# An attention, a dense layer and eight experts on one core: the first layer's tiles 0 and 1 begun inside the last pair of heads, and identity matmuls ahead of the first scores

## What is computed

```python
# attention over equal buckets, for 2 x 8 heads of 768 x 64
q_bucket = sum(((q @ proj) > 0) * powers)          # 6 bits; the same for k
scores = where(q_bucket == k_bucket, (q @ k.T) / 8, -1e9)
x = softmax(scores) @ v                            # -> 1536 tokens x 512
# first layer
h = maximum(x @ w_in, 0.0)                         # 512 -> 2048
x = (h * h) @ w_out                                # 2048 -> 512
# experts: w_gate gives logits; (token, expert) pairs are taken in order of size,
# at most 192 tokens for each of 8 experts; each token then goes through its expert
out[mask] = maximum(x[mask] @ w1[e], 0.0) @ w2[e]
```

## Time and profile before

| | us |
|---|---|
| median of 3 runs | 836.95 |
| lowest and highest | 836.59 and 838.42 |
| the profiled execution | 838.97 |
| its span, first to last instruction | 837.2 |
| TensorE busy | 783.4 (94%) |
| GpSimd busy | 398.9 (48%) |
| VectorE busy | 379.8 (45%) |
| ScalarE busy | 377.2 (45%) |

### The profile page before, as it was taken

How to read it: one execution, slowest core, us unless ns; L and a number is a source line. 1 busy time by engine, 2 the same in 40 slices (tenths; PEclk the granted TensorE clock), 3 DMA queues, 4 the chain that set the end, 5 groups by cost and what they waited for, 6 DMA issues and landing times. The chain is left out here.

```text
span 837.2 us, 14217 instructions
## 1 busy us (share of the span) xinstructions
PE 783.4 (94%) x4720; PEld 714.6 (85%) x4720; DVE 379.8 (45%) x875; ACT 377.2 (45%) x655; POOL 398.9 (48%) x326
## 2 busy tenths in 40 slices
PE   5999999999999799999999999984599999999986
PEld 3898898898887688999999999973499999999986
DVE  6576576576672443322232234224555345345500
ACT  2677777777676455545545554530012122212221
POOL 5567777777577576646656675640100110011001
PEclk9999999999999899999999999995599999999999
DMA  6564775875541000100000010010635455364541
GB/s 157 121 150 109 157 180 127 187 187 126 141 126 51 0 1 0 38 1 0 1 38 0 0 39 0 0 38 0 220 122 173 166 176 183 119 218 149 179 170 38
DMA packets 43687, 81.38 MB, mean 97 GB/s; under 512 B 17176, under 2 KB 17176, under 8 KB 43136
## 3 DMA queue, kind: packets, MB, share of 16 engines
q1 hardware_dynamic: 41440, 74.58, 31.5%
q0 software_dynamic: 2048, 6.29, 2.3%
q10 hardware_dynamic: 160, 0.00, 0.0%
HBM read 54.55 MB, written 6.29 MB: 73 GB/s over the span
## 5 line engine op out<-in xcount | busy, mean ns | idle before, releaser
L1122 PE MATMUL banks<-xt_hi,split_parts 128*128 128x384 f32 (+1 forms) x512 | 142.2, 339 | 0.2 <-POOL split_parts L886 0.2
L309 POOL TENSOR_TENSOR pt_lo<-pt,pt_hi 128x768 fp32r<-128x768 f32 x64 | 117.7, 1846 | 48.0 <-ACT pt_hi L438 38.4
L1133 PE MATMUL banks<-split_parts,h_hi 128*128 128x512 f32 x384 | 122.8, 401 | 5.7 <-DVE h_lo L1048 5.6
L886 POOL TENSOR_TENSOR split_parts<-w_in_sb,split_parts 128x512 fp32r<-128x512 f32 x64 | 84.4, 1319 | 91.1 <-ACT split_parts L879 89.8
L1045 DVE TENSOR_TENSOR h<-relu 128x384 f32<-128x384 f32 x64 | 43.6, 681 | 184.6 <-ACT relu L1000 184.6
L431 ACT ACTIVATE pt<-banks 128x768 f32<-128x768 f32 x96 | 78.1, 813 | 60.8 <-PE banks L683 54.2
L544 DVE TENSOR_REDUCE mx<-banks 128x1 f32<-128x768 f32 x96 | 90.5, 957 | 23.4 <-PE banks L710 19.5
L1566 PE MATMUL banks<-x_cols,w_in_sb 128*128 128x192 f32 x512 | 96.6, 342 | 1.1 <-ACT x_cols L1346 1.1
L1122 PEld LDWEIGHTS banks<-xt_hi,split_parts 128*128 128x128 f32 x512 | 94.3, 190 | 3.3 <-POOL split_parts L886 0.5
L1580 PE MATMUL banks<-expert_hidden,w_out_sb 128*128 128x192 f32 x512 | 94.0, 334 | 0.0
L890 POOL TENSOR_TENSOR split_parts<-w_out_sb,split_parts 128x512 fp32r<-128x512 f32 x64 | 84.2, 1315 | 16.2 <-ACT split_parts L882 16.2
(11 more groups left out here) (195 smaller groups left out, 1354.6 us busy)
## 6 DMA issues: line engine op xcount, KB each, us to landing
w_in_sb<-in_moe_w SPq DMA_DIRECT2D x8, 2048.0 KB, 9.7
w_out_sb<-in_moe_w SPq DMA_DIRECT2D x8, 2048.0 KB, 8.6
w_in_sb<-in_moe_w_in SPq DMA_DIRECT2D x8, 512.0 KB, 6.5
w_out_sb<-in_moe_w_out SPq DMA_DIRECT2D x8, 512.0 KB, 6.4
w_out_sb<-in_k SPq DMA_DIRECT2D x16, 192.0 KB, 3.7
w_out_sb<-in_q SPq DMA_DIRECT2D x16, 192.0 KB, 4.0
v_raw<-in_v SPq DMA_DIRECT2D x16, 192.0 KB, 3.4
ka<-split_parts SPq DMA_DIRECT2D x16, 192.0 KB, 3.0
```

The lines of the kernel that those rows point to most:

```text
L309: pool.tensor_tensor(pt_lo[x % 2][:], pt[j % 2][:], pt_hi[x % 2][:].bitcast(fp32), ALU.subtract).then_inc(los, 1)
L886: pool.tensor_tensor(wil[i], in_view(f), wih[i].bitcast(fp32), ALU.subtract).then_inc(wils, 1)
L1122: last = pe.matmul(PB[i][:, 0:HALF], w_[:, k, :], x_[:, xs], start=n == 0, stop=n == 3 * DT - 1)
L1133: last = pe.matmul(PB[2 + t][:], h_[:, tc], w_[:], start=start and n == 0, stop=stop and n == 2, skip_group_check=True)
```

## The change

It has these parts.

- The splits of the first weights go from the last pair of heads to the one before (`p + 2 == PAIRS`), spread between its steps. `weights(n)` runs for n = 2 to 9 (`w_in`) and 10 to 13 (`w_out`), one load in each half pair. ScalarE waits for nine loads, not twelve.
- `hidden` for tiles 0 and 1 goes into the last pair of heads on TensorE (`early_hidden`), behind `scores_t` 2 and 4 of head 15; relu and square (`tile`) stand in ScalarE's queue of the last pair.
- The last `sums`, `high`, `low` and `turn` of the attention go into the first layer's queues, behind or between its first steps (`later`).
- `project` does the products with high parts alone first, waits for the low part behind them, and `z_k`/`z_q` start on the high part.
- `keep_warm` on TensorE multiplies the identity by itself: nine matmuls of 128x384 before the first projection, three before `rows(0)`, four behind it.

```diff
-                if 4 <= n < 12:
-                    load_in(sp, n - 4)
-                if 9 <= n < 13:
-                    load_out(sp, n - 9)
+                if 2 <= n < 10:
+                    load_in(sp, n - 2)
+                elif 10 <= n < 14:
+                    load_out(sp, n - 10)
 # GpSimd, pair p
                     q_low(pool, p + 2)
+                if p + 2 == PAIRS:
+                    split["in_low"](pool, 0, 0, 0)
                 if p:
                     low(p - 1)
                 low_part(2 * p + 1, 1)
+                if p + 2 == PAIRS:
+                    split["in_low"](pool, 1, 1, 1)
                 low_part(2 * p + 1, 2)
+                if p + 2 == PAIRS:
+                    split["out_low"](pool, 0, 0, 0)
                 low_part(2 * p + 1, 3)
                 low_part(2 * p + 1, 4)
-                if p + 1 == PAIRS:
-                    split["in_low"](pool, 0, 0, 0)
-                    split["in_low"](pool, 1, 1, 1)
-                    split["out_low"](pool, 0, 0, 0)
...
-            low(PAIRS - 1)
+            later["low"] = lambda: low(PAIRS - 1)
 # ScalarE, pair p
-                if p + 1 == PAIRS:
-                    ...
-                    act.wait_ge(split["w_early"], 16 * 12)
-                    split["in_high"](act, 0, 0)
-                    split["in_high"](act, 1, 1)
-                    split["out_high"](act, 0, 0)
                 v_high(2 * p + 1, 1)
                 ...
                 q_high(p + 2)
+                if p + 2 == PAIRS:
+                    for taken in (ka_in, kb_in, qa_in, qb_in):
+                        act.wait_ge(taken[0], 32 * (PAIRS - 1) - (16 if taken in (kb_in, qb_in) else 0))
+                        act.wait_ge(taken[1], 32 * (PAIRS - 1))
+                    act.wait_ge(split["w_early"], 16 * 9)
+                    split["in_high"](act, 0, 0)
...
                 expo_high(2 * p + 1, 1)
+                if p + 2 == PAIRS:
+                    split["in_high"](act, 1, 1)
                 expo(2 * p + 1, 2)
                 expo_high(2 * p + 1, 2)
+                if p + 2 == PAIRS:
+                    split["out_high"](act, 0, 0)
...
                 expo(2 * p + 1, 4)
+                if p + 1 == PAIRS:
+                    split["tile"](act, 0, 0)
...
-            sums(HEADS - 1, 1)
-            high(PAIRS - 1)
+            split["tile"](act, 1, 1)
+            later["sums"] = lambda: sums(HEADS - 1, 1)
+            later["high"] = lambda: high(PAIRS - 1)
 # TensorE
-            def project(slot, hi, lo, done):
+            def project(slot, hi, lo, low, count, done):
                 for h in range(2):
                     c = slice(h * HALF, (h + 1) * HALF)
                     pe.matmul(slot[:, h, 0:HALF], p_hi[:], hi[:, c], start=True, stop=False)
-                    pe.matmul(slot[:, h, 0:HALF], p_hi[:], lo[:, c], start=False, stop=False)
-                    last = pe.matmul(slot[:, h, 0:HALF], p_lo[:], hi[:, c], start=False, stop=True)
+                    pe.matmul(slot[:, h, 0:HALF], p_lo[:], hi[:, c], start=False, stop=False)
+                pe.wait_ge(low, count)
+                for h in range(2):
+                    c = slice(h * HALF, (h + 1) * HALF)
+                    last = pe.matmul(slot[:, h, 0:HALF], p_hi[:], lo[:, c], start=False, stop=True)
...
+            def early_hidden(g):
+                if g == 0:
+                    pe.wait_ge(mxs, 6 * HEADS - 1)
+                    pe.wait_ge(xl, 5)
+                split["hidden"](pe, g, 0, g)
...
                 scores_t(2 * p + 1, 1, p, 2)
+                if last:
+                    early_hidden(0)
...
                 scores_t(2 * p + 1, 1, p, 4)
+                if last:
+                    early_hidden(1)
...
+            def keep_warm(slot, n):
+                for _ in range(n):
+                    pe.matmul(slot[:, 0, 0:HALF], identr[:], identr[:].unsqueeze(1).broadcast_to([P, 3, P]), start=True, stop=True)
+
+            keep_warm(PREP, 9)
             pe.wait_ge(proj_split, 1)
...
+            pe.wait_ge(mxs, 5)
+            keep_warm(PREP, 3)
             rows(0, 0)
+            keep_warm(PREP, 4)
             pair(0, 1, True, False)
 # first layer, GpSimd
             for g in range(6):
                 both_low(g, g + 2, g + 1, g % 2)
+                if g == 1:
+                    later["low"]()
 # first layer, ScalarE, first chunk
+                    in_high(2, 2, 0)
+                    out_high(1, 1, 1)
+                    later["sums"]()
+                    in_high(3, 3, 1)
+                    out_high(2, 2, 0)
+                    later["high"]()
                     for g in range(2, 8):
                         tile_high(g, g + 2, g + 1, g % 2)
 # first layer, VectorE, first chunk: tile j
                     hidden(c * FT + j, j % 2)
                     if first:
-                        if j == 1:
+                        if j < 2:
+                            later["divisors"](j)
+                        elif j == 3:
 # first layer, TensorE
-            hidden(0, 0, 0)
             chunk(0, 0, HALF, True, False)
```

More of the change, by code:

```diff
@@ L639, in _, with last_divisors @@
             pair(PAIRS - 1, 0, False, True)
[L641 to L644, removed]
+            def last_divisors(h):
+                turn(HEADS - 1, 1, h)
+                if h:
+                    reciprocals(HIGH)
+            later["divisors"] = last_divisors
         @block.tensor
@@ L839, in _ @@
             weigh_low(HEADS - 1, 1, 4, False, True)
+        return later
 def routing_constants(nc, ctx):
@@ L870, in weight_splits, with hidden, tile @@
     wihs, wils, wohs, wols = (sem("split_" + n) for n in ("wihs", "wils", "wohs", "wols"))
+    hid, relus, hhs = (sem("first_" + n) for n in ("hid", "relus", "hhs"))
+    r32 = [ctx.enter_context(nc.sbuf_tensor(f"relu{i}", [P, HALF], fp32)) for i in range(2)]
+    hh = [ctx.enter_context(nc.sbuf_tensor(f"h_hi{i}", [P, HALF], f32r)) for i in range(2)]
+    def hidden(pe, g, x0, i):
+        pe.wait_ge(wils, g + 1)
+        n = 0
+        for k in range(DT):
+            xs = bass.ds(x0 + k * S, HALF)
+            for w_, x_ in ((wih[i], xt_hi), (wih[i], xt_lo), (wil[i], xt_hi)):
+                last = pe.matmul(PB[i][:, 0:HALF], w_[:, k, :], x_[:, xs], start=n == 0, stop=n == 3 * DT - 1)
+                n += 1
+        last.then_inc(hid, 1)
+    def tile(act, g, i):
+        act.wait_ge(hid, g + 1)
+        act.activation(r32[i][:], PB[i][:, 0:HALF], ACT.Relu).then_inc(relus, 1)
+        act.wait_ge(relus, g + 1)
+        act.activation(hh[i][:], r32[i][:], ACT.Square).then_inc(hhs, 1)
     def in_view(f):
@@ L892, in weight_splits, with first_layer @@
     return dict(stage=stage, wih=wih, wil=wil, woh=woh, wol=wol, wihs=wihs, wils=wils, wohs=wohs, wols=wols, w_early=w_early, w_ready=w_ready,
-                in_high=in_high, out_high=out_high, in_low=in_low, out_low=out_low)
-def first_layer(nc, block, sem, PB, ident, K, finish, low_done, xt_hi, xt_lo, split, wg, L, stored, y_rows):
+                hid=hid, relus=relus, hhs=hhs, r32=r32, hh=hh, hidden=hidden, tile=tile, in_high=in_high, out_high=out_high, in_low=in_low, out_low=out_low)
+def first_layer(nc, block, sem, PB, ident, K, finish, low_done, xt_hi, xt_lo, split, wg, L, stored, y_rows, later, h32, hl):
     with ExitStack() as ctx:
@@ L1108, in _ @@
         def _(pe):
-            pe.wait_ge(split["w_early"], 16 * 12)
-            pe.wait_ge(split["w_ready"], 16 * 5)
+            pe.wait_ge(split["w_early"], 16 * 9)
+            pe.wait_ge(split["w_ready"], 16 * 8)
             pe.sem_inc(rows_done, 2)
             def hidden(g, x0, i):
-                pe.wait_ge(wils, g + 1)
-                if past(g, 2):
-                    pe.wait_ge(relus, g - 1)
-                n = 0
-                for k in range(DT):
-                    xs = bass.ds(x0 + k * S, HALF)
-                    for w_, x_ in ((wih[i], xt_hi), (wih[i], xt_lo), (wil[i], xt_hi)):
-                        last = pe.matmul(PB[i][:, 0:HALF], w_[:, k, :], x_[:, xs], start=n == 0, stop=n == 3 * DT - 1)
-                        n += 1
-                last.then_inc(hid, 1)
+                pe.wait_ge(relus, g - 1)
+                split["hidden"](pe, g, x0, i)
             def rows(g, i, start, stop):
@@ L1189, in chunk @@
                 if not last:
-                    pe.wait_ge(head_low, 1)
+                    if not first:
+                        pe.wait_ge(head_low, 1)
                     hidden(g0 + FT, x_next, 0)
@@ L1227, in experts @@
             K["weigh"], K["ones"], K["tri"], K["iota_j"], K["tabs"], K["masks"], K["lift"], K["pref"], K["ids"])
+        xg = [sb(f"x_rows{i}", [CH, 2, DM]) for i in range(2)]
+        xgt = sb("x_cols", [P, DT, CAP])
+        hs = sb("expert_hidden", [P, F2T, CAP])
+        oc = sb("expert_out_cols", [P, DT, CAP])
+        og = sb("expert_out", [CH, 2, DM])
         m = sb("best", [P, NT])
```

49 lines of the change are left out of this document (19 added, 30 removed).

## The result

| | before | changed |
|---|---|---|
| median of the runs, us | 837.32 (836.59 to 838.42, 4 runs) | 829.3 (827.04 to 830.64, 4 runs) |
| ratio | | 0.9889, 95% interval 0.9851 to 0.9927 |
| the profiled execution, its span | 838.97, 837.2 | 830.64, 828.9 |

The forecast was 829.9. The span fell by 8.3 us, where the terms of the forecast gave 7.1. The total is close. The reason given for its largest term was in good part not right, and one gain of 1.0 us has no term in it.

The account below looks back on a forecast made before the run. TensorE was taken as the bound: only its idling, low clock or added work counts. From 838.97 us, -8.8 (passage and pair 6) and +1.7 (front) give 831.9, less 2.0 for the median: 829.9; range 827.2 to 833.8.

Parts of the forecast that it names:

- What bounds the kernel: Whole kernel: TensorE is busy throughout full stretches, so time is lost only to its idling, lower clock or added work.
- Passage, 8.6 us removed: From attention to first layer: 0.20 and 5.63 us idle plus 2.75 us of low clock go, with h_lo ready.
- Filling the last pair, 1.3 us: Last pair of heads: the moved hidden groups fill part of its 1.45 us of TensorE idle time, gaining 1.3 us.
- New stalls, 0.8 us: First layer's start: hidden group 2 and rows group 2 wait on late GpSimd and VectorE steps, costing 0.8 us.
- Pair 6, 0.3 us: Pair 6: moved splits delay GpSimd's third low part of head 13 by about 1.1 us, costing 0.3 us.
- Weights' loads, nothing: Attention pairs: weights' loads, one each half pair from pair 1 instead of two from pair 2, cost nothing.
- The front, +1.7 us: Kernel start: warming gains 0, opens a gap of some 3 us before head 1's scores; the fallen clock costs 1.7 us.
- High parts first, nothing: Projections inside the loop: TensorE is full and low parts are ready long before, so the new order gains 0.
- A: Front: the clock holds through the gap; 828.2 us, or 827.5 with all gaps of the last pair filled; 25%.
- B: Passage and pair 6: new waits on GpSimd and VectorE queues replace the old one; 832.9 to 834.2 us; 20%.
- C: Attention from 29 us: the clock stays at 1.2 GHz, a whole pair giving 843.7 us, slower than before; 3%.
- D: Last pair: hidden group 0 waits inside it as long as it did behind it; 837 to 838 us; 2%.

Follow-up runs that it names:

- the kernel with hidden 0 and 1 behind: Changed kernel with the first two hidden groups after the attention's last matmul and their relu and square after its last exponential; 830.86 us.
- the kernel with the early splits alone: Kernel before with only the first weights' splits and the loads they need moved to pair 6; 830.9 us, ratio 0.99.
- the kernel with the filled gap: Changed kernel with fifteen more identity matmuls behind weigh(0, 0, 0), ahead of the scores of head 1; 825.38 us, ratio 0.9833.
- the one with the wait for the low part: Changed kernel with later q loads, no identity matmuls, and z_k and z_q waiting for the low part before their first matmul; 828.02 us.
- The front alone: Kernel before with only project, z_k, z_q and keep_warm of the changed kernel; 838.81 us, ratio 1.0012.

## Why the prediction came out right, step by step

One row of the trace of before bears on the first of the terms, the last `sums` of the attention on ScalarE:

```profile
273.98 0.81 ACT L448 ACTIVATE num<-banks 64x768 f32<-64x768 f32 x1 [6.66 <-POOL inverse L316]
```

- **What bounds the kernel.** Right: all that was won was idle time, low clock or (the layer's pace) length of TensorE's own work.
- **Passage, 8.6 us removed.** Right in size: no gap, no low clock. By the starts of TensorE's matmuls 9.1 us went: the last two of the attention to rows group 5 took 34.78 us (268.47 to 303.25) and now take 22.45 (273.48 to 295.93); 4.17 of the difference are the two moved groups, and 0.96 of new stalls (below) stand against the rest. The reason given was right in part: it named the attention's last `sums` and `high` ahead of the relu in ScalarE's queue. But it said that the gap goes because hidden 0 gets a head start in the last pair, and with hidden 0 behind the pair there was no gap either. The gap came from the order in two queues, and the forecast overlooked the first of them. GpSimd's three subtractions stood ahead of the divisions, ScalarE's `sums` waited for these, and the relu stood behind that (the earlier trace rows has the subtractions at 268.16, the divisions at 271.88 and VectorE's wait for the relu until 276.20; the row above has the 6.66 us that `sums` waited for the divisions). Out of the 9.1 us the passage gave at rows group 5, moving the splits to pair 6 gives 5.3, letting the attention's last steps go behind the first tiles' relu 3.0 (the difference to the kernel with hidden 0 and 1 behind), and the head start 0.7. The 9.1 is firm: less their lateness behind pair 6, the seven executions of kernels with all these parts reach rows group 5 9.0 to 9.1 us earlier than before.
- **Filling the last pair, 1.3 us.** The last two matmuls of the attention start at 268.47 in before. With the lateness of 1.74 and two hidden groups of 2.08 each (half of the changed kernel's 4.17 for a tile) they would start at 274.38 without a fill. They started at 273.48: 0.9 us. About half of it is the copies' departure, since the kernel with the early splits alone also got 0.46 us less late in this pair.
- **New stalls, 0.8 us.** Hidden 2 waited 0.50 for the row that was named, at the top of its 0.2 to 0.5; rows 2 came 0.17 late and rows 3 0.07. Together 0.74; by the starts, rows 0 to rows 3 take 13.47 us, 0.96 more than three tiles at 4.17. The price of VectorE's steps behaved as said: 1.49 us at 275.64 beside GpSimd at work, 0.56 at 273.84 in the kernel with hidden 0 and 1 behind, where GpSimd had nothing to do. The Trainium skill, "SBUF — State Buffer", section "SBUF: two separate sides", says that such a VectorE step and such a GpSimd instruction take one port pair in turn; this case's trace agrees (1.49 and 0.56 us).
- **Pair 6, 0.3 us.** 0.35 by the marks. The third low part was 1.0 us later than the lateness carried in, as forecast 1.1.
- **Weights' loads, nothing.** Right for the profiled execution: the lateness stays between 1.39 and 1.55 us from the first pair to the sixth. Other executions of kernels with the new loads show a wait for a transfer in the attention (last section).
- **The front, +1.7 us.** The mechanism was right: the scores stayed, a gap of 3.23 us opened, the clock fell and came back after 3.4 us. The cost was 1.5 us, of which the runs put 1.1 on the clock; 0.4 is that the queue's own end came later with the warming (29.13 to 29.46 in five executions, against 28.91 and 28.94 where TensorE waited without it). TensorE's work ahead of the gap ended at 26.05, where 25 to 26 was forecast, though the clock was down from 15.1 to 21.9 (last section). The Trainium skill, "TensorE: Matmul & The Clock Gate", section "HAM oscillation — how this bites in real kernels", tells of a kernel in which such a wait for a load between two bursts throttled the clock again; the trace agrees (0.50 behind 28.7), and the kernel with the filled gap shows the price.
- **High parts first, nothing.** Right for this kernel. With the queue's bound moved away the first scores of head 1 came 0.87 us earlier, of which 0.25 us are the early start's own.
- **What had no term.** The layer's pace, 1.0 us. The sum was -8.8 + 1.7 = -7.1. Measured at rows group 5: -9.1 + 0.35 + 1.4 (the front at the last mark ahead of pair 6) = -7.3; with the pace -8.3, which is the span's difference. That the part behind the layer took the same 282.9 us in both executions is chance, by the spread told above.
- **The rivals.** A (the clock holds) didn't happen in the changed kernel and did where the gap was 0.32, 1.55 or 1.94 us; its 827.5 isn't what its terms give, all 1.45 us filled make 828.0. B's waits were there at a third of its price, 0.96 us of 3.0. C: the clock came back within the first pair. D: hidden 0 ran at 261.49 without a wait.

The experiments point to a faster version: with the loads of q later (826.08, or 825.18 without warming) or with the gap filled (825.38). All three medians lie below the changed kernel's 829.3 and 830.16; the intervals of the ratios overlap a little with its own, and it is the marks, 1.1 to 2.9 us earlier than in the changed kernel at the first and 1.4 to 2.8 at the last rows group, that show the gain. Which of the three is best the medians don't tell.

## What to carry to other kernels

When an engine waits, follow the releaser back through every queue to the first instruction that stands in the wrong place, and try that move alone: here three subtractions on GpSimd ahead of two divisions held TensorE, by way of ScalarE and VectorE. Warming an engine that then waits for a transfer only moves the idle time to the place just ahead of the full load; look first for what sets the next start (here one queue of transfers), and move that. Whether warming pays then wasn't shown here. And compare two kernels by marks of the same work within an execution: they told 1.1 us of clock and 1.0 us of pace where medians scatter by more. Take more than one execution of each, and read the clock beside the marks: a wait for a transfer or a clock that rises 1.6 us later moves a mark by 0.6 us as well.

## What the runs showed of the hardware

- The place of buffers in SBUF changed the length of matmuls: 397 against 395 ns as a mean over some 330 that read `h_hi`, 395 in both for those that read `h_lo`. It is 0.02 us for each tile of 4.18, 1.0 us over the layer, the same in every kernel with either placement. Which buffer does it, and why, is open.
- The clock fell in or just behind gaps of 2.40 (early splits), 3.17, 3.23, 3.28 and 3.39 us; it held through gaps of 0.32, 0.55, 1.55 and 1.94 us ahead of the same work. The one of 1.17 us in the earlier trace rows was followed by light work and a fall 2.3 us later. In the changed kernel the same work behind a like wait saw no fall (the clock is 1.00 from 598.8 to 796.7), so the gap alone isn't the whole story:

```profile
708.22 0.88 PE L1590 MATMUL banks<-ident,x_rows 96*128 96x96 f32 x8 [1.13 <-DMA x_rows<-y_rows,token_list]
```

- The clock can fall without a long gap. During the first scores, where each pair of matmuls waits for a row maximum, it went down at 15.1 us in the changed kernel in spite of the nine identity matmuls ahead. In the kernel with the filled gap, with the same code and the same waits of 0.24 us up to here, it stayed at 1.00. So the same stretch can go either way:

```profile
14.42 0.62 PE L723 MATMUL banks<-kb,qb 128*128 128x384 f32 x2 [0.25 <-DVE mx L552]
...
15.28 1.01 PE L723 MATMUL banks<-kb,qb 128*128 128x384 f32 x2 [0.24 <-DVE mx L552]
```

- A transfer can cost TensorE 0.5 to 1.0 us at a place where another execution shows nothing. In the kernel without warming the scores at 104.15 wait for the one-row transfer from `kb` to `qb`; SyncE issued it at 101.24, and its next issue took 1.55 us in place of some 0.5:

```profile
101.24 0.54 SPq L211 DMA_DIRECT2D qb<-kb  x1
101.82 1.55 SPq L183 DMA_DIRECT2D ka<-xt_lo  x1
...
104.15 0.96 PE L723 MATMUL banks<-kb,qb 128*128 128x384 f32 x4 [0.80 <-DMA qb<-kb]
```

The same wait, 0.70 to 0.97 us, is at that place in the three kernels with early splits and in the one with the wait for the low part, and not in before or in the changed kernel. The front alone has one of 0.53 us at 197.85, and the repeat of the changed kernel the one of 0.48 at 61.98, where its first execution has none. So it isn't tied to one edit, nor to every execution of one kernel. Its cause is open; whether the earlier loads of the weights make it likelier is open too (five of the eleven executions with them have it at 104, neither of the two without). It is also why 0.7 us up or down between two of these kernels, in a median or in a later mark, says little of the edit itself.
